# A convolution and two feed-forward layers on one core: the low parts of x wait for another semaphore, taps and drain are reordered

## Time and profile before

| what | us |
|---|---|
| median of 3 runs (1474.7 to 1476.08) | 1474.76 |
| the profiled execution | 1475.9 |
| its span, first to last instruction | 1474.1 |
| TensorE busy | 1295.3 (88%) |
| VectorE busy | 1102.5 (75%) |
| ScalarE busy | 1084.7 (74%) |
| GpSimd busy | 362.2 (25%) |
| mean granted clock of TensorE | 0.929 |

### The profile page before, as it was taken

One profiled execution on the slowest core, in us unless ns is written; L12 is line 12 of the kernel. 1 busy time (PEld: TensorE's weight loads), 2 busy tenths in 40 slices (PEclk: granted clock), 3 DMA queues, 4 the chain that ended last, 5 costly groups with the idle time before them and its releaser, 6 DMA issues.

```text
span 1474.1 us, 26101 instructions
## 1 busy us (share of the span) xinstructions
PE 1295.3 (88%) x10722; PEld 1140.8 (77%) x10722; DVE 1102.5 (75%) x973; ACT 1084.7 (74%) x1128; POOL 362.2 (25%) x180
## 2 busy tenths in 40 slices
PE   7998789976999669996699876998869987799999
PEld 4767578865989569885698866987769876798988
DVE  7996489964899548994599945998559976488840
ACT  7987578964888558885588765887658966689853
POOL 3432122212222212212122222222122221222200
PEclk9999899998999879998799987999879998799999
DMA  6110000010000100000000010000000000000000
GB/s 207 37 22 1 1 4 9 5 31 0 12 1 12 23 1 12 1 12 23 1 12 1 12 23 0 12 1 29 6 0 12 1 12 1 1 12 1 12 1 22
DMA packets 14825, 21.64 MB, mean 15 GB/s; under 512 B 1792, under 2 KB 9984, under 8 KB 14592
## 3 DMA queue, kind: packets, MB, share of 16 engines
q1 hardware_dynamic: 14576, 20.01, 4.7%
q10 hardware_dynamic: 144, 0.01, 0.0%
HBM read 13.72 MB, written 6.29 MB: 14 GB/s over the span
## 4 chain that ended last, share of the span: by engine, by line
PE 48%; issue 24%; DVE 14%; ACT 6%; POOL 6%; DMA 1%; SPq 0%; ACTq 0%; POOLq 0%; DVEq 0%
PE o L665 11%; PE h L637 10%; PE h L643 9%; PE o L649 8%; POOL gl L445 4%; PE o_tail L655 4%; DVE work L1086 3%; DVE work L1092 2%; DVE work L1125 2%; DVE work L1118 2%; PE o L505 2%; DVE work L1089 2%; ACT work L860 2%; ACT work L896 1%; POOL x_lo L374 1%
## 5 line engine op out<-in xcount | busy, mean ns | idle before, releaser
L445 POOL TENSOR_TENSOR gl<-work,gh 128x1024 fp32r<-128x1024 f32 x126 | 301.6, 2394 | 617.1 <-ACT gh L869 568.5
L1086 DVE SCALAR_TENSOR_TENSOR work<-work,coef,h 128x1024 f32<-128x1024 f32 x128 | 163.8, 1279 | 285.1 <-ACT work L860 284.8
L665 PE MATMUL o<-v,work 64*128 64x192 f32 x3584 | 359.4, 336 | 0.0
L665 PEld LDWEIGHTS o<-v,work 64*128 64x128 f32 x3584 | 338.8, 197 | 12.2
L950 ACT ACTIVATE work<-work,coef 128x1024 f32<-128x1024 f32 x128 | 146.5, 1144 | 211.2 <-POOL gl L445 211.2
L649 PE MATMUL o<-gh,v_hi 64*128 64x512 f32 x448 | 154.8, 427 | 122.4 <-POOL gl L445 120.4
L859 ACT ACTIVATE work<-h,coef 128x1024 f32<-128x1024 f32 x128 | 154.2, 1205 | 109.7 <-PE h L637 105.2
L649 PEld LDWEIGHTS o<-gh,v_hi 64*128 64x128 f32 x448 | 85.6, 200 | 141.7 <-issue 137.5
L637 PE MATMUL h<-x_hi,w_hi 64*128 64x512 f32 x448 | 140.8, 449 | 34.0 <-POOL x_tail L430 34.0
L1129 DVE SCALAR_TENSOR_TENSOR work<-work,coef 128x1024 f32<-128x1024 f32 x128 | 164.5, 1285 | 4.5
L1092 DVE SCALAR_TENSOR_TENSOR work<-work,coef,h 128x1024 f32<-128x1024 f32 x128 | 164.0, 1281 | 4.5
(11 more groups left out here) (142 smaller groups left out, 2948.9 us busy)
## 6 DMA issues: line engine op xcount, KB each, us to landing
out_dram<-y_out SPq DMA_DIRECT2D x32, 192.0 KB, 2.0
xt<-in_x_main_dram SPq DMA_DIRECT2D x7, 518.0 KB, 4.8
xt_tail<-in_x_tail_dram SPq DMA_DIRECT2D x8, 259.0 KB, 5.4
work<-in_moe_w_out_dram SPq DMA_DIRECT2D x2, 768.0 KB, 9.1
v<-in_moe_w_out_dram SPq DMA_DIRECT2D x1, 1536.0 KB, 7.5
raw_w_tail_late<-in_moe_w_in_dram SPq DMA_DIRECT2D x4, 256.0 KB, 6.5
work<-in_moe_w_in_dram SPq DMA_DIRECT2D x2, 512.0 KB, 6.4
xt<-in_x_main_dram SPq DMA_DIRECT2D x2, 259.0 KB, 7.1
```

Of the source, the lines that this page charges most:

```text
L445: nc.gpsimd.tensor_tensor(gl[:, j % 2, :], r_buf[j % 2], gh[:, j % 2, :].bitcast(F32), ALU.subtract).then_inc(gl_ready, 1)
L665: last = pe.matmul(o2[:, bank, c, 0:D], g2[buf_out][rows, col:col + P], v2[rows, f, :], start=(f == 0 and c == 0 and turn == 0), stop=(f = ...
L1086: nc.vector.scalar_tensor_tensor(q_buf[buf], w_of_n, b0_abs, h_flat, ALU.add, ALU.mult).then_inc(z_done, 1)
```

## The change

Four edits:

- The four low parts of x on GpSimd wait for `w_ready` at n + 1 (ScalarE has done L860 of unit n) in place of `g_ready` at n (VectorE has done g of unit n - 1).
- `A_MAIN` moves from unit (1,5) to (1,4). The two copies of the first tile's tail change their order: the raw copy to the lower rows (which the subtraction overwrites) is now in unit (1,6) behind L939, the high part to the upper rows in (1,7) ahead of L859.
- The taps: main taps 0 to 6 in (0,0), (0,1), (0,3), (0,5), (0,6), (0,7), (1,0), tail taps in (0,3), (1,1) two, (1,3) three, (1,5). They are done behind the unit's other work on VectorE. The first main tap waits for three of the four low parts of the pair, no longer for all four.
- In the drain TensorE does, in each step, first the second product of layer 1 (in the second step those of two units), then the second product of layer 2, and then the first product of layer 2. Before, the first product of layer 2 came first, and the second product of layer 1 mostly last.

```diff
-    TAPS_AT = {(0, 1): (("pair", 0), ("tail", 0)), (0, 3): (("pair", 1),), (0, 5): (("pair", 2), ("tail", 1)),
-               (0, 6): (("pair", 3),), (0, 7): (("pair", 4), ("tail", 2)), (1, 0): (("pair", 5),),
-               (1, 1): (("pair", 6), ("tail", 3)), (1, 3): (("tail", 4), ("tail", 5)), (1, 5): (("tail", 6),)}
+    TAPS_AT = {(0, 0): (("pair", 0),), (0, 1): (("pair", 1),), (0, 3): (("pair", 2), ("tail", 0)),
+               (0, 5): (("pair", 3),), (0, 6): (("pair", 4),), (0, 7): (("pair", 5),), (1, 0): (("pair", 6),),
+               (1, 1): (("tail", 1), ("tail", 2)), (1, 3): (("tail", 3), ("tail", 4), ("tail", 5)),
+               (1, 5): (("tail", 6),)}
...
                7: (("pair_b", (3, 4, 5, 6)),), 8: (("tail", (0, 1, 2)),), 9: (("tail", (3, 4, 5, 6)),)}
-    A_MAIN, A_TAIL = (1, 5), (1, 7)
+    A_MAIN, A_TAIL_RAW, A_TAIL = (1, 4), (1, 6), (1, 7)
     B_MAIN, B_TAIL = (0, 0), (0, 1)
     FIRST_SECOND_SPLIT = 3
...
             def low_of_x(pair, batch, n):
                 pool.wait_ge(x1_hi_ready, counted(pair * 4 + 2 * batch + 1))
-                pool.wait_ge(g_ready, counted(n))
+                pool.wait_ge(w_ready, counted(n + 1))
                 nc.gpsimd.tensor_tensor(x1_lo[batch][:, :], conv[:, batch, :], x1_hi[batch][:, :].bitcast(F32),
                                         ALU.subtract).then_inc(x1_lo_ready, 1)
...
                         low_of_x(i + 1, 0, n)
                     if tile(t) and pair_exists(i + 1) and (parity, j) == A_TAIL:
                         pool.wait_ge(x1_tail_copied, counted(i + 1))
-                        pool.wait_ge(g_ready, counted(n))
+                        pool.wait_ge(w_ready, counted(n + 1))
                         rows = x1_tail[0][LOWER, :]
                         nc.gpsimd.tensor_tensor(rows, conv_tail[LOWER, :], rows.bitcast(F32),
                                                 ALU.subtract).then_inc(x1_lo_ready, 1)
...
                         pool.wait_ge(x1_hi_ready, counted(i * 4 + 4))
                         pool.wait_ge(gl_ready, counted(n - 2))
                         pool.wait_ge(x1_lo_ready, counted(i * 4 + 3))
-                        pool.wait_ge(g_ready, counted(n))
+                        pool.wait_ge(w_ready, counted(n + 1))
                         nc.gpsimd.tensor_tensor(x1_tail[1][LOWER, :], conv_tail[UPPER, :],
                                                 x1_tail[1][UPPER, :].bitcast(F32), ALU.subtract).then_inc(x1_lo_ready, 1)
                         pool.wait_ge(x1_lo_ready, counted(i * 4 + 4))
...
             def second_product_of_layer_1(n, j, t):
                 k = (j - OUT1_LAG) % UNITS
-                if k == 0:
+                if k == 0 and tile(t):
                     pe.wait_ge(x2_lo_ready, counted(t))
                     pe.wait_ge(x2_sum_ready, counted(t))
                     if first(t):
...
                         last.then_inc(colsum_ready, 1)
                     if early:
                         conv_of_unit(n)
+                    if not tile(t):
+                        if j < OUT1_LAG - 1 and unit(n - OUT1_LAG):
+                            second_product_of_layer_1(n, j, t)
+                        second_product_of_layer_2(t, j, m, k2)
+                        if j == OUT1_LAG - 2 and unit(n - OUT1_LAG):
+                            second_product_of_layer_1(n + 1, j + 1, t)
                     if unit(m):
                         if k2 == 0:
                             pe.wait_ge(w_hi_ready, 13)
...
                             pe.wait_ge(t3_done, n)
                         x2p = (parity + (j - SKEW) // UNITS) % 2
                         first_product_of_layer_2(k2, x2p, t2)
-
-                    ends_layer_1 = not tile(t) and j == OUT1_LAG - 1
-                    if not tile(t) and not ends_layer_1:
-                        second_product_of_layer_2(t, j, m, k2)
-                    if unit(n - OUT1_LAG):
+                    if tile(t) and unit(n - OUT1_LAG):
                         second_product_of_layer_1(n, j, t)
-                    if ends_layer_1:
-                        second_product_of_layer_2(t, j, m, k2)
             run(pe, phase)
...
                         act.wait_ge(h1_ready, counted((i + 1) * 2 * UNITS - UNITS))
                         nc.scalar.copy(x1_hi[0][:, :], conv[:, 0, :]).then_inc(x1_hi_ready, 1)
                     if tile(t) and pair_exists(i + 1) and (parity, j) == A_TAIL:
                         tail_convolved(i + 1)
-                        nc.scalar.copy(x1_tail[0][LOWER, :], conv_tail[LOWER, :]).then_inc(x1_tail_copied, 1)
+                        nc.scalar.copy(x1_tail[0][UPPER, :], conv_tail[LOWER, :]).then_inc(x1_hi_ready, 1)
                     if tile(t) and later_pair(i) and (parity, j) == B_MAIN:
                         act.wait_ge(h1_ready, counted(i * 2 * UNITS))
                         nc.scalar.copy(x1_hi[1][:, :], conv[:, 1, :]).then_inc(x1_hi_ready, 1)
...
                         act.wait_ge(u_ready, counted(m))
                         act.wait_ge(out2_done, counted(m - 2))
                         nc.scalar.activation(g2[buf], u_relu, ACT.Square).then_inc(g2_ready, 1)
-                    if tile(t) and pair_exists(i + 1) and (parity, j) == A_TAIL:
-
-                        nc.scalar.copy(x1_tail[0][UPPER, :], conv_tail[LOWER, :]).then_inc(x1_hi_ready, 1)
+                    if tile(t) and pair_exists(i + 1) and (parity, j) == A_TAIL_RAW:
+                        tail_convolved(i + 1)
+                        nc.scalar.copy(x1_tail[0][LOWER, :], conv_tail[LOWER, :]).then_inc(x1_tail_copied, 1)
                     if ahead(n + 1) and n > 0:
                         act.wait_ge(t3_done, 1 if n == 1 else n + 1)
...
                 x_k, w_k, dst = xt[:, tiles, k:k + TOK], cw[:, 0, k:k + 1], conv[:, tiles, :]
                 if k == 0:
                     dve.wait_ge(x_loaded, counted(pair * 32))
-                    dve.wait_ge(x1_lo_ready, counted(pair * 4))
+                    dve.wait_ge(x1_lo_ready, counted(pair * 4 - 1))
                     ins = nc.vector.tensor_scalar(dst, x_k, w_k, None, ALU.mult)
                 else:
                     dve.wait_ge(main_step, counted(step))

```

## The result

The changed kernel took 1259.15 us (median of 4 runs, 1257.08 to 1259.84) against 1475.01 us before in the same series. The ratio is 0.8533, 95% interval 0.8518 to 0.8548. The forecast was 1243.6, its range 1232 to 1275: the direction and most of the size held, 15.5 us of the gain did not come. The profiled execution (1258.79 us) has a span of 1257.0 us.

The account below looks back on a forecast made before the run. Bound: low parts of x, waiting for the previous unit's g, delay `gl` and L950 28 times. Gains of 198.6 (six periods), 13.7, 16.9 and 2.0 make 231.2 us off 1474.76: 1243.6 us, range 1232 to 1275.

Parts of the forecast that it names:

- The new wait: At four low-part places: low part ends +3.6, `gl` +6.0, L950 0.1 us late per place, bounds 0 and 0.5.
- The second rival: GpSimd and VectorE block each other at the 28 low-part places: 1256 us, up to 1311; chance 0.11.
- A period: 16 units: 12 plain at 9.00, two layer-2 split stretches at 19.36, small extras; 147.7 us against 180.81.
- the third tail tap: At (1,3), three tail taps instead of two put 0.5 us a period on the path.
- the raw copy: At (1,6), between L939 and L950 on ScalarE: cost 0.1 us a period, bounds 0 and 0.6.
- Tap 0: At +0.82 of (0,1), GpSimd idle: taken under 1.0 us, hidden; at 2.93 it would cost 1.4 a period.
- The border: At (0,0): the 34.0 us of `x_tail` waits go too, not counted again; TensorE itself is late next.
- The clock: TensorE's granted clock is 1.00 from one end of the kernel to the other.
- The third rival: TensorE stays at the lower clock: gain eaten up from 27 of 128 units, 1588 us with 40; chance 0.03.
- The sum of six periods: The gain of one period, 33.1 us, taken six times: 198.6 us.
- Head, tail, drain: Gains before the first full period 13.7 us, in the last period 16.9, in the drain 2.0.
- The range: Own range 1232 to 1262 us, extended to 1275 to take in the lower part of the GpSimd-VectorE blocking case.

Follow-up runs that it names:

- experiment 1: The kernel before with the three new waits alone; taps, copies, A_MAIN and drain as before: 1261.94 us, ratio 0.8552.
- experiment 2: The changed kernel with its three waits put back to g, all else kept: 1477.88 us, ratio 1.0013.
- experiment 7: The changed kernel with the low parts waiting for VectorE's third step on h instead of ScalarE's second: 1399.93 us, ratio 0.947.
- experiment 3: The changed kernel with TensorE's hardware loop over pairs 1 to 6 written out, other engines keeping theirs: 1241.02 us, ratio 0.8411.
- experiment 5: The kernel before the change with TensorE's loop written out: 1475.79 us, ratio 0.9995.

## Why the prediction was right, and where it was not, by its own steps

- **The new wait.** Right to 0.1 us at three of the four places: low part to +3.57 (said +3.6), `gl` to +5.97 (+6.0), L953 0.15 late (0.1). At (1,4) the low part was as long as the longest that the prediction allowed for (1.73 us, said 1.71 at most) and `gl` ended at +6.4. That the late wait was all of the stall is shown by experiments 1 and 2 together.
- **The second rival** came at no cost that shows. At three places it missed by a narrow margin: L1122 starts when `gl` ends. At (1,4) GpSimd and VectorE did meet, through a tap that the prediction had not set beside the low part, but another wait ended later. The sign set for this rival, L1118 (now L1122) later than +6.2 where a low part lies, says little at (1,4): an output step stands ahead of it there, and it went from +7.01 to +7.48, the lateness of the tap. Experiments 2 and 7 show that the mechanism exists. With the low parts 3.8 us later in the unit the kernel is 141 us slower, of which the expectation gave 112 - 16 = 96 to the lateness alone.
- **A period.** Said 147.7, measured 146.83 where there is no jump: the split of layer 2's input cost 9.06 + 10.02 = 19.08, not 19.36, twice; the third tail tap 0.40 (said 0.5), the raw copy 0.13 (0.1), the four places nothing that shows. Tap 0 took 0.75 us with GpSimd idle, not the estimated 0.55, and was hidden as said.
- **The border, the step that failed.** The prediction said that TensorE's 34.0 us of waiting for `x_tail` lie inside the stretched units and that behind them "what is late next is TensorE itself", at 9.00 a unit. But under that wait lay the loop's jump back, which costs 2.4 to 3.9 us and had been free. Five jumps, 16.3 us: experiments 3 and 5. The profile before held a sign that I did not use: TensorE's stream was known to be a loop, and no row showed the border without another wait on top.
- **The clock.** Said 1.00 from one end to the other. Over the first units (18.06 to 147.07) it is 0.96. From there on it is 1.00 but for three of the five jumps, where 2 us of idle time are followed by work at the lower level (0.59 over 293.3 to 297.5); behind the two others, with as much idle time, it stays at 1.00. The third rival did not come.
- **The sum of six periods.** I took one period, 180.81 us, six times. The six lie between 160.09 and 1242.34 and take 1082.25, so 180.4 each: the forecast was 2.6 us too low by that alone.
- **Head, tail, drain.** Three units ahead of the first full period 28.7 (said 28.5), four behind it 37.16 (37.4), drain 1.8 (2.0).
- **The range.** Two of its sums are a little off: 28 x 0.4 is 11 and not 12, so the second rival begins at 1255, and the upper end by its own terms is 1263. That 1259 lies in the range is partly luck: the range went above 1243.6 for late low parts, a slow tap 0 and the second rival, and the 15.5 us came from something that no term of it held.

Span by these terms: 1242.9 + 16.3 + 2.6 - 6 x 0.87 = 1256.6, against 1257.0.

## What to carry to other kernels

A helper instruction on an engine with much idle time is not free: what counts is what stands behind it in its queue, so let it wait for the earliest event that is safe, not for a late one, and look at what the other engine runs beside it then. Before a large wait is taken out, ask what else happens at the same spot in the stream, a loop's jump among it, for its cost appears when the wait is gone. And a sum over repeated stretches should use their total, not one of them times their number.

## What the runs showed of the hardware that I had not expected

- At a jump back of its loop TensorE was idle for 2.13 to 2.27 us, five times of five. Two of five units grew by 2.4 us, three by 3.8 to 3.9, which ran on at the lower clock level behind the gap.
- In experiment 7, at (1,7), VectorE's L1129 was held over two GpSimd instructions in a row (4.49 us for 1.22): the next one in GpSimd's queue went ahead of the instruction that was waiting. At (0,0) and (0,1) the waiting L1129 came through between the two (2.17 to 2.20 us). What decides which goes first stays open.
- The first unit starts at 16.2 to 16.5 us in the three kernels with TensorE's loop written out, at 17.67 with all loops written out, and at 16.94 to 18.06 in those that keep it, one execution of each. No row says why.
